# Batch 0's gates, odd low splits and reciprocals leave VectorE, and its dense stage starts two slots earlier

## The reference

```python
scores = q @ k.T / 8; kth = 32nd largest of each row
attn = softmax(where(scores >= kth, scores, -1e9)); x = attn @ v      # heads side by side: 576 x 512
gate = sigmoid(causal 5-tap convolution of x along the tokens, one weight per tap and channel)
x = (gate * (x @ w_val)) @ w_out
u = x + real(fft over tokens and channels of x)
out = u + relu(layernorm(u) @ w_ch1) @ w_ch2                          # w_ch1: 512 x 2048
```

## Time and profile before

| | |
|---|---|
| median of 3 runs | 1170.51 us |
| the profiled execution's own time | 1171.51 us |
| its span | 1169.7 us |
| granted TensorE clock, mean of the span | 0.945 |
| busy: TensorE, VectorE, ScalarE, GpSimd | 1037.2, 876.2, 617.2, 403.8 us |

### The profile page before, as it was taken

One profiled execution on the slowest core, in us unless ns is written; L12 is line 12 of the kernel. 1 busy time (PEld: TensorE's weight loads), 2 busy tenths in 40 slices (PEclk: granted clock), 3 DMA queues, 4 the chain that ended last, 5 costly groups with the idle time before them and its releaser, 6 DMA issues.

```text
span 1169.7 us, 19830 instructions
## 1 busy us (share of the span) xinstructions
PE 1037.2 (89%) x6608; PEld 827.9 (71%) x6608; DVE 876.2 (75%) x1901; ACT 617.2 (53%) x1253; POOL 403.8 (35%) x703
## 2 busy tenths in 40 slices
PE   3776666589999999999989999999889999999998
PEld 2455555576577888866578888875678888648887
DVE  6999999997998897897998987897988960220000
ACT  3776775555556665644566756555566654012211
POOL 2444452223443422332443423233453222233221
PEclk9987666699999999999999999999999999999999
DMA  7655556011256675620367775411367555207974
GB/s 218 216 179 189 171 175 219 21 31 57 68 186 217 242 259 207 205 67 21 114 220 255 250 231 190 155 57 52 139 221 248 207 205 198 95 1 287 342 273 164
DMA packets 81188, 200.37 MB, mean 171 GB/s; under 512 B 8384, under 2 KB 26560, under 8 KB 81088
## 3 DMA queue, kind: packets, MB, share of 16 engines
q1 hardware_dynamic: 80928, 198.81, 50.3%
q10 hardware_dynamic: 160, 0.30, 0.1%
HBM read 177.58 MB, written 21.50 MB: 170 GB/s over the span
## 4 chain that ended last, share of the span: by engine, by line
PE 39%; issue 27%; POOL 14%; DVE 12%; ACT 4%; DMA 2%; SPq 1%; POOLq 0%; DVEq 0%; ACTq 0%
PE p_m L490 12%; PE p_m L596 10%; PE p_m L582 10%; DVE rest L780 5%; POOL hid_lo L995 3%; DVE top L786 3%; PE p_t L463 2%; POOL bias L931 2%; PE p_t L479 2%; POOL bias L930 2%; PE p_s L450 2%; ACT prob L663 2%; DMA u<-w_ch 1%; POOL x_new L942 1%; POOL q_st L919 1%
## 5 line engine op out<-in xcount | busy, mean ns | idle before, releaser
L786 DVE MAX8 top<-rest 128x8 f32<-128x576 f32 x432 | 304.7, 747 | 0.0
L780 DVE MATCH_REPLACE8 rest<-top,rest 128x576 f32<-128x576 f32 x288 | 211.7, 743 | 0.0
L995 POOL TENSOR_TENSOR hid_lo<-hid,hid_hi 128x256 fp32r<-128x256 f32 (+1 forms) x128 | 104.7, 818 | 303.6 <-ACT hid_hi L725 303.6
L596 PE MATMUL p_m<-w_st,hid_hi 128*128 128x512 f32 x640 | 202.3, 397 | 1.5 <-POOL hid_lo L995 1.5
L582 PE MATMUL p_m<-un_hi,w_st 128*128 128x320 f32 (+1 forms) x1024 | 165.9, 304 | 13.4 <-ACT hid_hi L725 9.6
L663 ACT ACTIVATE prob<-s_sb,bias 128x576 f32<-128x576 f32 x144 | 111.1, 772 | 108.0 <-POOL bias L931 107.8
L463 PE MATMUL p_t<-id_sb,prob 128*128 128x128 f32 x720 | 118.8, 300 | 52.1 <-ACT prob L668 29.9
L582 PEld LDWEIGHTS p_m<-un_hi,w_st 128*128 128x128 f32 x1024 | 143.1, 189 | 26.5 <-issue 23.6
L656 ACT ACTIVATE s_sb<-p_s 128x576 f32<-128x576 f32 x144 | 93.0, 646 | 95.0 <-PE p_s L450 94.8
L479 PE MATMUL p_t<-pT,v_sb 128*64 128x128 f32 (+1 forms) x1600 | 111.5, 292 | 33.9 <-issue 17.8
L450 PE MATMUL p_s<-k_hi,q_st 128*128 128x512 f32 (+1 forms) x320 | 116.2, 366 | 24.2 <-ACT s_sb L656 14.5
(11 more groups left out here) (84 smaller groups left out, 1581.9 us busy)
## 6 DMA issues: line engine op xcount, KB each, us to landing
w_st<-w_split SPq DMA_DIRECT2D x256, 512.0 KB, 4.5
w_split<-w_st SPq DMA_DIRECT2D x32, 512.0 KB, 3.0
k_raw<-kT SPq DMA_DIRECT2D x62, 144.0 KB, 3.0
q_raw<-qT SPq DMA_DIRECT2D x60, 144.0 KB, 2.9
u<-w_ch SPq DMA_DIRECT2D x32, 256.0 KB, 3.4
v_sb<-v SPq DMA_DIRECT2D x16, 256.0 KB, 3.7
wslot<-w_val SPq DMA_DIRECT2D x4, 1024.0 KB, 5.4
wslot<-w_out SPq DMA_DIRECT2D x4, 1024.0 KB, 5.4
```

The source lines that it names most:

```text
L596: mm = pe.matmul(mbank(j), h[i % 2][:, P * j:P * j + P], w2_st[i % NB2][:, w, :], start=f == 0 and part == 0, stop=f == FC - 1 and part == 2)
L780: dve.match_replace(rest[tt % 2][:, :], top[tt % NK][:, 8 * n - 8:8 * n], src[:, :], LOWEST).then_inc(s_chain, 1)
L786: found = dve.max(top[tt % NK][:, 8 * n:8 * n + 8], rest[tt % 2][:, :])
L995: pool.tensor_tensor(hid_lo[i % 2][:, 0:WIDTH[g]], hid[:, 0:WIDTH[g]], hid_hi[i % 2][:, 0:WIDTH[g]].bitcast(F32), ALU.subtract).then_inc(m ...
```

## The change

It does the following at once.

- **Reciprocals** of all tiles go from VectorE to GpSimd, at the head of the odd slots, ahead of `biases`; the reciprocal itself becomes a power of -1.
- **Odd low splits** of pairs 1 to 4 (slots 6, 15, 24, 33) go from VectorE to GpSimd, at the slot's end.
- **Batch 0's convolution** goes from VectorE to TensorE: GpSimd makes 20 diagonal matrices in slots 11 to 14, and each channel block is two groups of five products of 288 columns, in slots 15, 17, 24, 26, 33, 35, 41 and 41; ScalarE's Tanh then reads the PSUM banks (slots 18, 27, 36, 41).
- **Tile 35**, the last of batch 0, is attended in slot 41 instead of 42, behind tile 34, with `store_out` and `scale_out` of both ahead of `exponent` and `biases` there.
- **Six value products** follow in slot 41; the other steps are spread over slots 42 to 78.
- **VectorE** runs the steps of slots 41, 42 and 43 in its own slots 39, 40 and 42.

The diff, cut to its core (constants, semaphores and the batch-0 conditions that only follow from it are left out):

```diff
+EARLY = NT - 1
+HURRY = EARLY + TRANSPOSE
+HURRY_STEPS = 6
+SOONER = {HURRY: HURRY - 2, HURRY + 1: HURRY - 1, HURRY + 2: HURRY + 1}
+POOL_PAIRS = PAIRS
+CONV_BANK = [1, 2]
+DIAG_AT = {11: 0, 12: 1, 13: 2, 14: 3}
+CONV0_AT = {15: (0, 0), 17: (0, 1), 24: (1, 0), 26: (1, 1), 33: (2, 0), 35: (2, 1), HURRY: (3, 1)}
+TANH0_AT = {18: 0, 27: 1, 36: 2, HURRY: 3}
...
+        n = 0
+        if b == 0:
+            start, n = HURRY + 1, HURRY_STEPS
+            out[HURRY] = steps[0:n]
...
+        def attended(s):
+
+            tiles = [s - ATTEND] if due(s, ATTEND) and unit_end(s - ATTEND) is not None and s - ATTEND != EARLY else []
+            return tiles + ([EARLY] if s == HURRY else [])
...
+                def convolve(c, o):
+
+                    pe.wait_ge(s_x, 5 * c + (5 if o else 3))
+                    if o == 0:
+                        pe.wait_ge(s_diag, TAPS * (c + 1))
+                        if c:
+                            pe.wait_ge(m_tanh, c)
+                        else:
+                            pe.wait_ge(s_feat_ev, KC)
+                    for k in range(TAPS):
+                        mm = pe.matmul(mbank(CONV_BANK[o], HALF_S), diag(c, k),
+                                       x_new[c][:, k + o * HALF_S:k + o * HALF_S + HALF_S], start=k == 0, stop=k == TAPS - 1,
+                                       skip_group_check=True)
+                    if o:
+                        mm.then_inc(s_conv, 1)
...
@@ TensorE, in each slot @@
-                    for x in plan[s][0:1]:
+                    for x in first_steps(s):
                         step(*x)
-                    if unit_due(s):
-                        attend(s - ATTEND)
-                    for x in plan[s][1:]:
+                    for t in attended(s):
+                        if t == EARLY:
+                            convolve(KC - 1, 0)
+                        attend(t)
+                    if s in CONV0_AT:
+                        convolve(*CONV0_AT[s])
+                    for x in other_steps(s):
                         step(*x)
...
@@ VectorE, in each slot @@
-                    if due(s, RECIP) and (s - RECIP) % 2:
-                        reciprocal(s - RECIP)
...
-                    if split_at(s, LOW0, LOW) and split_at(s, LOW0, LOW)[1] == 1:
-                        split_low(split_at(s, LOW0, LOW)[0])
+                    p, h = split_at(s, LOW0, LOW) or (0, 0)
+                    if p > POOL_PAIRS and h == 1:
+                        split_low(p)
...
-                    for x in plan[s]:
-                        step(*x)
+                    for at in plan:
+                        if SOONER.get(at, at) == s:
+                            for x in plan[at]:
+                                step(*x)
...
@@ GpSimd @@
+                def split_low_odd(p):
+                    pool.wait_ge(s_hi, 5 * (p + 1))
...
+                    for to, of in ((slice(0, whole), slice(0, whole)), (slice(whole + REST, SP), slice(whole, S))):
+                        pool.tensor_tensor(q[0:D, to], q_in[0:D, of], q[0:D, to].bitcast(F32),
+                                           ALU.subtract).then_inc(s_lo[1], 1)
+                    pool.tensor_tensor(k[:, :], k_in, high[:, :].bitcast(F32),
+                                       ALU.subtract).then_inc(s_lo[1], 1)
...
+                def reciprocal(t):
+
+                    pool.wait_ge(s_exp, t + 1)
+                    if t >= NK:
+                        pool.wait_ge(s_pv, unit_of(t - NK) + 1)
+                    c = slice((t - 1) % NK, (t - 1) % NK + 2)
+                    pool.tensor_scalar(rinv[:, c], psum_row[:, c], EPS_SUM, 2.0, ALU.add, ALU.mult).then_inc(s_radd, 1)
+                    pool.wait_ge(s_radd, t // 2 + 1)
+                    pool.tensor_tensor(rinv[:, c], rinv[:, c], power[:, 1:3], ALU.pow).then_inc(s_rinv, 1)
...
+                def make_diags(c):
+                    pool.wait_ge(s_resid, 80)
+                    pool.wait_ge(s_const, 16)
+                    for k in range(TAPS):
+                        pool.tensor_scalar(diag(c, k), id_sb[:, :], cw_sb[:, c, k:k + 1], None, ALU.mult).then_inc(s_diag, 1)
...
@@ GpSimd, in each slot @@
+                    if due(s, RECIP) and (s - RECIP) % 2:
+                        reciprocal(s - RECIP)
+                    if s == HURRY:
+                        for t in attended(s):
+                            scale_out(t)
                     if due(s, EXPONENT):
                         biases(s - EXPONENT)
                     if part_due(s) is not None:
                         split_weights(part_due(s))
...
+                    if s in DIAG_AT:
+                        make_diags(DIAG_AT[s])
```

More of the change, by code:

```diff
@@ L99, in steps_by_slot @@
         steps = [(what, b, n) for what, n in STEPS]
-        start = NT * (b + 1) + ATTEND
+        start, end = NT * (b + 1) + ATTEND, NT * (b + 2) + ATTEND
         if b == B - 1:
@@ L104, in steps_by_slot @@
             break
[L105 to L109, removed]
+        n = 0
+        if b == 0:
+            start, n = HURRY + 1, HURRY_STEPS
+            out[HURRY] = steps[0:n]
+        total = sum(COST[x[0]] for x in steps[n:])
+        spent = 0.0
+        for i in range(start, end):
+            while n < len(steps) and spent + COST[steps[n][0]] / 2 <= total * (i + 1 - start) / (end - start):
+                out[i].append(steps[n])
                 spent += COST[steps[n][0]]
                 n += 1
-        out[start + NT - 1] += steps[n:]
+        out[end - 1] += steps[n:]
     return out
@@ L139, in build @@
         id_sb = sb("id_sb", [P, P])
-        power = sb("power", [P, 1])
+        power = sb("power", [P, 3])
         q_raw = sb("q_raw", [P, S])
@@ L278, in split_at, with first_steps, other_steps @@
             return (p + 1, h) if h is not None and p + 1 < ALL_PAIRS else None
-        def unit_due(s):
-            return due(s, ATTEND) and unit_end(s - ATTEND) is not None
+        def attended(s):
+            tiles = [s - ATTEND] if due(s, ATTEND) and unit_end(s - ATTEND) is not None and s - ATTEND != EARLY else []
+            return tiles + ([EARLY] if s == HURRY else [])
+        def first_steps(s):
+            return [] if s == HURRY else plan[s][0:1]
+        def other_steps(s):
+            return plan[s] if s == HURRY else plan[s][1:]
         def split_due(s):
@@ L290, in conv_due @@
         def conv_due(s):
-            return [(b, c, taps) for b in range(B) for c, taps in CONV_AT.get(s - NT * b, [])]
+            return [(b, c, taps) for b in range(1, B) for c, taps in CONV_AT.get(s - NT * b, [])]
         def tanh_due(s):
-            return [(b, TANH_AT[s - NT * b]) for b in range(B) if s - NT * b in TANH_AT]
+            return [(b, TANH_AT[s - NT * b]) for b in range(1, B) if s - NT * b in TANH_AT]
         def part_tile(i):
@@ L512, in values @@
                         pe.wait_ge(m_gv, upto_gv(b, j - 3))
+                    elif j == 2 and b == 0:
+                        pe.wait_ge(m_tanh, KC)
                     n0, n1 = VAL[half]
@@ L803, in split_low @@
                                       ALU.subtract).then_inc(s_lo[1], 1)
[L805 to L813, removed]
                 def conv(b, c, taps):
```

68 lines of the change are left out of this document (45 added, 23 removed).

## The result

The changed kernel takes 1220.4 us (median of 4 runs, 1219.9 to 1222.3) where the kernel before took 1171.4 us beside it: a ratio of 1.042, with a 95% interval of 1.0405 to 1.0436. The direction was as forecast. The size was not: +49 us instead of +14, outside the range of 1162 to 1200.

A forecast was written before the change was run, and what follows sets the result against it. The prediction took a closed loop of ScalarE and GpSimd to bound the front and TensorE the rest; 23.8 - 9.5 + 0.8 + 2.9 - 4 = +14.0 us gave a median of 1184 us, range 1162 to 1200.

The forecast's parts named there:

- The mechanism: In the front, ScalarE and GpSimd run a closed loop; VectorE, relieved, gains some 6 us before waiting for it.
- The first rival: VectorE alone limits the front, so selection of tile 35 ends 29.7 us sooner: 1132 to 1164 us, chance 0.2.
- the second: Half of the loop's growth hides in the turns' room, last rounding near 195: 1165 to 1176 us, chance 0.18.
- The loop's growth L: Up to slot 33's weight rounding, the ScalarE-GpSimd loop gets longer by 23.8 us.
- The diagonals: Twenty products of 128 columns on GpSimd in slots 11 to 14: 0.33 us each, 6.6 us (4.4 to 9.2).
- the 5 us "hidden": Up to slot 33, GpSimd's added work finds 5 us of room in turns bound by ScalarE and TensorE.
- the sum's 3.8 us: TensorE's convolution lengthens the turns of slots 17 and 26, 5.9 and 5.7 us otherwise, by 3.8 us together.
- The convolution's turns: A loop turn with a TensorE convolution lies between 6.1 and 12.1 us; taken at 7.7.
- The third rival: Convolutions run at TensorE's low clock, six turns of up to 12.1 us: 1210 us at most, chance 0.07.
- `exponent` 28 to 35: This stretch, 44.8 us when paced by VectorE's convolution, takes 35.3 us, so -9.5 us.
- From there to the first value product: From `exponent` 35, through slot 41, to the first value product: 13.5 us instead of 12.7, +0.8 us.
- Behind the first value product: Two slots' scores and transposes still ahead on TensorE add 2.9 us; VectorE's relief halves TensorE's idle time, -4 us.

The follow-up runs named there:

- e1: The changed kernel with ScalarE's weight rounding ahead of `exponent` in each slot; 1199.1 us, 1.0241.
- e5: The changed kernel with the twenty diagonal products back on VectorE; 1210.2 us, 1.0331.
- e4: As e3, with all reciprocals back on VectorE; 1193.3 us, 1.0186.
- e3: The changed kernel without the six value products in slot 41 and without VectorE's earlier steps; 1212.6 us, 1.0352.
- e6: The changed kernel with the odd low splits of pairs 1 to 4 back on VectorE; 1215.3 us, 1.0378.
- e13: The changed kernel with reciprocals, odd splits and diagonals on VectorE and no early dense steps, loop closed; 1175.5 us, 1.0035.
- e10: The changed kernel with the reciprocals of tiles from 36 on (slot 43 and later) back on VectorE; 1210.2 us, 1.0338.
- e14: As e13, with batch 0's convolution back on VectorE, leaving tile 35 in slot 41 and steps in slots 42 to 78; 1179.5 us, 1.0068.
- e15: As e16, with batch 0's reciprocals on GpSimd and the later ones left on VectorE; 1163.9 us, 0.993.
- e16: The kernel before with odd splits of pairs 1 to 4 on GpSimd and weight rounding ahead of `exponent` from slot 8 on; 1170.5 us, 0.9993.
- e9: The kernel before with all reciprocals alone moved to GpSimd; 1182.9 us, 1.0106.
- e11: As e4, with weight rounding ahead of `exponent`; convolution on TensorE, diagonals and odd splits on GpSimd stay; 1177.9 us, 1.0049.
- e8: As e13, with ScalarE's weight rounding ahead of `exponent`; 1175.1 us, 1.0032.

## Why the prediction was wrong in size

Against the profiled execution of before the span grew by 50.9 us, where the sum had 14.0. By the sum's own steps:

1. **The mechanism** (closed loop, VectorE would wait): right, shown by e1, and by the 43.9 us that VectorE waits for ScalarE's copies (10 to 25 were forecast up to 240 us). The first rival, VectorE alone at the limit, fell with that; so did the second, since the last rounding lay not near 195.
2. **The loop's growth L**: forecast +23.8, measured 218.14 - 183.71 = +34.4. In the sum two terms carry the difference of 10.6. The diagonals were taken at 0.33 us each, between bounds of 0.22 and 0.46; they took 0.62 (twenty of them 12.3 us instead of 6.6: +5.7), outside both. And the 5 us "hidden" are not seen in the sum: GpSimd's 29.4 us more left its wait as it was. Single parts behave differently. At slot 33 the diagonals gave back 13.0 us of 12.3 (e5), the reciprocals 11.8 of 15.3 (e4 against e3), the odd splits 2.95 of 8.9 (e6). So some of the work does hide (the split of slot 15), and some is offset, since splits on VectorE make other turns longer. In exchange the convolution costs more than the sum's 3.8 us: e13, which has it without GpSimd's work, is 5.1 us late at slot 33, and ScalarE's wait for TensorE's scores grew by 10.3 us. The power took 0.73 us on its two columns instead of 0.56, and a reciprocal with its gaps 1.09 us (89.71 to 90.80) instead of 0.95, 2.0 us more over fourteen; that is offset among the smaller terms. By the trace the odd split (1.55 and 1.42 us from 111.44 us on, forecast 2.9 together) and the bias's relief (418 to 302 ns, as forecast) were right. One reading was off without effect: the selection of tile 35 ended at 215.4 us in the kernel before; 216.5 is where the next pair begins.
3. **The convolution's turns** of 7.7 us: measured 7.5, 7.7, 8.6 and 7.7 in slots 15, 17, 24 and 26. The third rival would have had them at up to 12.1, at the low clock. The mean of the stretch, 0.72 (0.74 before), hides what counts, the clock in these four turns:

```profile
109.23:116.74 7.51, 5.43 (x27) 4.19 (x25) 3.07 (x6) 3.63 (x9) 4.96 (x7) 0.94 0.44 137
122.18:129.90 7.72, 5.75 (x29) 4.20 (x25) 5.59 (x10) 4.24 (x10) 2.22 (x4) 0.90 0.47 142
164.13:172.75 8.62, 4.79 (x26) 3.78 (x24) 6.39 (x14) 3.64 (x10) 5.90 (x9) 0.93 0.48 158
177.11:184.78 7.67, 5.69 (x31) 4.25 (x27) 2.85 (x7) 4.28 (x10) 3.13 (x6) 0.92 0.55 176
```

   It is 0.90 to 0.94, near the upper of the two levels, and one matmul instruction of 288 columns took 0.41 us in the median of 80 (two for each product). So the third rival fell. The Trainium skill (TensorE: Matmul & The Clock Gate, HAM oscillation) has pauses between bursts put the array back to its low rate, and the prediction read it as the case to expect. In these turns the trace does not agree with that reading. e13, where the same turns take 11.3, 7.6, 5.6 and 5.6 us, is 4 us slower than before, not 26.
4. **`exponent` 28 to 35**: forecast 35.3 us, measured 36.3 (216.50 to 252.84). **From there to the first value product**: forecast 13.5, measured 13.5. These two steps stood.
5. **Behind the first value product**: forecast +2.9 - 4 = -1.1, measured 50.9 - 26.8 = +24.1. This is the step that failed most. Two parts of it are shown. The reciprocals of the later tiles cost 10.2 us (e10, 1.0 of it already there at the first value product); the sum costed only the fourteen up to slot 33, though the change moves all 72, and took for granted that what leaves VectorE in a TensorE-bound stage is a gain. And the early start costs 7.8 us (e3), where the text let the gate wait cost "up to 8 us" but put it at nothing and gave VectorE's relief 4 us. The wait is 19.58 us against 13 forecast. Together these are 18 of the 25.2 us by which this step was off; no run shows the rest. TensorE is busy 43.4 and 42.3 us of the windows from 300 and 350 us, where it had 46.4 and 47.4 before, though on work of a different place in the program.

Taken apart by experiments, the 49 us are: reciprocals 19.3 (e4 against e3), diagonals 10.2 (e5), odd splits 5.1 (e6), early start 7.8 (e3), and 4.7 for what is left in e13: 47.1. That they nearly add at the end is in part chance: at slot 33 they are not carried alike, as said above. Tile 35's place with the steps from slot 42 on costs 8.7 by itself (e14) and the convolution gives 4 of it back. One thing open: the reciprocals can hardly stay on VectorE beside its earlier steps, since in slot 39 it would wait for value products that need reciprocals it has not made; that combination was not run, and for the same reason the changes are not independent.

## What to carry to other kernels

Before time is moved to an engine that idles, see what it idles for: if its wait is for an engine that itself waits for it, the idle time is part of a loop and holds nothing; the wait did not shrink by 1 us under 29 us of work. Then look whether the order of one queue closes the loop: moving one step ahead of another was worth 21 us in the loaded kernel and nothing in the unloaded one, so the order is to be tried together with the work. And cost a moved instruction over the whole kernel, not only over the stretch for which it was moved: the reciprocals behind batch 0 alone cost 10.2 us (e10). In e15, with the loop open and only batch 0's moved, they bring 6.6 us (against e16); in e9, with the loop closed and all 72 moved, they cost 12. Last, see what an opened loop makes wait in its place: VectorE's reciprocals waited 18.7 us for ScalarE in e11.

## What was unexpected of the hardware

GpSimd was slower on one input than on two. The diagonals' durations (min, median, max in ns, first and last start):

```profile
L1033 POOL TENSOR_SCALAR un<-id_sb,cw_sb x8: 602/618/627, 78.6 to 95.7; 128x128 f32<-128x128 f32 x8
L1033 POOL TENSOR_SCALAR u<-id_sb,cw_sb x8: 599/606/632, 96.3 to 105.1; 128x128 f32<-128x128 f32 x8
```

The two-input `x_new` of the same size took 0.45 us in slot 12 above. From the 1.03 cycles an element of the Trainium skill (GPSIMD Engine Reference, Elementwise — side-by-side cycle accounting) the prediction had estimated 0.3; no run agrees with that for this form, whose multiplier is a column with one value for each partition.

The same instruction on VectorE takes 0.275 us in the median, but five times that beside GpSimd's two-input subtractions. In e8, by duration:

```profile
L888 DVE TENSOR_SCALAR un<-id_sb,cw_sb x8: 265/275/426, 72.5 to 83.9; 128x128 f32<-128x128 f32 x8
...
L888 DVE TENSOR_SCALAR ab<-id_sb,cw_sb x4: 270/1359/1504, 68.3 to 71.2; 128x128 f32<-128x128 f32 x4
```

GpSimd's timeline of e8 over the same 68.3 to 72.5 us:

```profile
68.46 1.27 POOL L1036 TENSOR_TENSOR w_st<-u,w_st 128x512 fp32r<-128x512 f32 x1 [1.08 <-ACT w_st L750]
69.69 1.40 POOL L997 TENSOR_TENSOR q_st<-q_raw,q_st 64x576 fp32r<-64x576 f32 x1
71.06 1.44 POOL L1000 TENSOR_TENSOR k_lo<-k_raw,k_hi 128x576 fp32r<-128x576 f32 x1
```

The four products took VectorE 4.25 us together instead of 1.1, while GpSimd's 1.27 to 1.44 us are what they are elsewhere. In the kernel before it is the other way round: GpSimd's one-column bias, 0.30 us in the median, took 1.65 us beside VectorE's two-input odd split, whose 0.80 and 0.75 us are its usual ones. GpSimd's line and VectorE's:

```profile
88.52 1.65 POOL L931 TENSOR_SCALAR bias<-top 128x1 f32<-128x1 f32 x1
```

```profile
88.61 0.80 DVE L800 TENSOR_TENSOR q_st<-q_raw,q_st 64x512 fp32r<-64x512 f32 x2
89.33 0.75 DVE L802 TENSOR_TENSOR k_lo<-k_raw,k_hi 128x576 fp32r<-128x576 f32 x1
```

So in both places it was the instruction with one tensor input that was slowed beside the other engine's two-input ones, whichever engine it was on.
